# Stage 2 of a fused attention and feed-forward kernel: gate and value products by Strassen's method

## The chip, the cores and the metric

The kernel runs on one core of one Trainium2 chip. The metric is the device time of one execution in microseconds (us), as the median of several runs; lower is better.

## What is computed

Three layers in a row, all in 32-bit floats:

```python
attn_out = _attn_ref(q, k, v, n_global, n_local)       # 2 batches, 8 heads, 768 tokens, 64 per head
x = attn_out.transpose(0, 2, 1, 3).reshape(1536, 512)
h = x @ w_in                                           # 512 to 1024
solu = h * softmax(h)
y = (solu - mean) / sqrt(var + 1e-6) * g_ln @ w_out    # 1024 to 512
xn = y / sqrt(mean(y * y) + 1e-6) * rms_g
g, val = xn @ w_gate, xn @ w_val                       # 512 to 1536, each
out = (g / (1 + exp(-g)) * val) @ w_down               # 1536 to 512
```

The attention looks at 8 global keys and at the 96 keys before each query. The last three lines are stage 2.

## The kernel before, in words

**Precision.** Each matrix product is made of three matmuls (`product`, L412 to L415): every operand is split into a rounded part `hi` (ACT rounds it by a copy) and a rest `lo` (DVE subtracts), and hi*hi, hi*lo and lo*hi are summed in PSUM. So each weight and each activation costs one instruction on ACT and one on DVE besides the matmuls.

**Attention and first feed-forward.** The 1536 tokens go in 12 tiles of 128 (`one_tile`, t from -1 to 11), each with four slots p = 0 to 3, one for each pair of heads. Each engine runs its own hand-written list of one tile after another (PE from L1371, ACT from L762, DVE from L1129, POOL from L647, SP from L508), and the order on an engine is the order in which these functions call the operations. Semaphores tie the lists together. While tile t+1 is attended, tile t runs through `ffn_in` in slots 1 and 2, and tile t-1 is normalised: DVE takes the variance at slot 0 of the next tile (`take_variance`, L1059), POOL works out the inverse root by ten tiny instructions, each waiting for the last (`newton`, L582), DVE applies it at slot 1 (`apply_norm`, L1077), and PE turns the result at slot 2 (`turn_ln`, L1297) and multiplies by `w_out` (`ffn_out`, L1311). ACT copies y out and squares it (`copy_y`, L713), and SP stores it to a spill buffer in HBM (L438).

**Stage 2.** Tokens go in 6 blocks of 256 in the outer loop, and each block passes all 1536 hidden columns in 12 steps m of 128. All weights of stage 2 lie split in SBUF for the whole stage. A block's y is loaded (`load_y`, L442), scaled by an inverse root from POOL (`newton_y`, L604; DVE L1088 and L1103), turned on PE (`turn_y`, L1325), and split by ACT and DVE (L723, L1112). In a step (`one_step`, L1412) PE makes a gate product and a value product (`widen`, L1342: 4 k x 3 matmuls of 128 x 256 each), then the down product of the step before (`narrow`, L1355: 2 x 3 matmuls of 128 x 512), which is summed over all 12 steps in two PSUM banks. ACT takes the SiLU and rounds, DVE multiplies and splits (L735, L741, L1121, L1126). After the last step of a block ACT copies the two banks out and SP stores them (`copy_out`, L743; `store_out`, L453).

**Around the seam.** The weights of stage 2 are brought in and split by a table of slots (L399 to L408) while the last tiles are attended. After tile 11 PE does the rest of `ffn_out` of tile 10, three steps of stage 2 with `turn_ln` of tile 11 between them, and then all of `ffn_out` of tile 11 (L1459 to L1468). POOL's list there is `newton(t)` for every tile, with `newton_y(0)` after `newton(8)` and the others at the end (L647 to L654).

## Time and profile before

| what | value |
|---|---|
| median of 3 runs | 592.25 us (591.99 to 592.34) |
| the profiled execution, its own time | 591.57 us |
| span of its profile, first to last instruction | 589.8 us |
| TensorE clock granted, mean over the span | 0.991 of full |
| PE busy in the span | 558.5 us (95%), 3697 matmuls |
| DVE, ACT, POOL busy | 307.1, 265.5, 93.9 us |

PE is TensorE, DVE is VectorE, ACT is ScalarE, POOL is GpSimd, SP is SyncE, which issues the DMAs here. A matmul's shown duration is longer than its distance to the next one, since matmuls overlap in the array: prices of a matmul are taken from start to start. Lines "L..." are lines of the kernel before.

### The profile page before, as it was taken

To read this page: it belongs to the slowest core of one execution; us is meant where nothing else is said; L and a number is where in the kernel's file an instruction comes from. 1 tells how busy PE (TensorE), PEld (TensorE's weight loads), DVE (VectorE), ACT (ScalarE), POOL (GpSimd) and SP (SyncE) were. 2 spreads that over 40 slices of the span, in tenths; PEclk is the share of its full clock that TensorE was granted. 3 is DMA by queue.
4 is the path that set the end of the run, shared out by engine and by line. 5 is a ranking of instruction groups with operands and counts; after the bars stand their busy time and mean duration, and the time that the engine had idled before them with its cause. 6 is when DMAs were issued, how large, how long until landed. Compare 5 with 4: busy or idle time off the path is not lost.

```text
span 589.8 us, 10771 instructions
## 1 busy us (share of the span) xinstructions
PE 558.5 (95%) x3697; PEld 480.2 (81%) x3697; DVE 307.1 (52%) x790; ACT 265.5 (45%) x610; POOL 93.9 (16%) x223
## 2 busy tenths in 40 slices
PE   2786999999999999999999999999999999999997
PEld 1564777777777777768899999999999999999996
DVE  4769878877887898767465132222212222222221
ACT  3668666776677786746443212222221222222112
POOL 4541122124202223323000010000001000000000
PEclk9997999999999999999999999999999999999999
DMA  8656662444244422414340200020020000001000
GB/s 216 193 148 183 198 174 77 125 125 125 76 125 125 127 76 76 159 57 176 111 170 9 73 1 1 1 72 0 1 72 0 0 0 36 0 0 37 1 1 36
DMA packets 21613, 46.95 MB, mean 80 GB/s; under 512 B 2764, under 2 KB 2776, under 8 KB 21576
## 3 DMA queue, kind: packets, MB, share of 16 engines
q1 hardware_dynamic: 21264, 46.47, 26.2%
q8 instruction: 20, 0.33, 0.2%
q14 instruction: 17, 0.14, 0.1%
q10 hardware_dynamic: 312, 0.01, 0.0%
HBM read 40.18 MB, written 6.29 MB: 79 GB/s over the span
## 4 chain that ended last, share of the span: by engine, by line
PE 80%; DVE 10%; POOL 4%; issue 3%; ACT 1%; DMA 1%; ACTq 0%; DVEq 0%; SPq 0%
PE hidden L413 9%; PE hidden L414 8%; PE hidden L415 8%; PE mixed L1265 3%; PE turned L413 3%; PE turned L414 3%; PE mixed L413 3%; PE scores_a L413 3%; PE mixed L414 3%; PE scores_b L413 3%; PE scores_a L414 3%; PE scores_b L414 3%; PE scores_b L415 3%; PE scores_a L415 3%; PE turned L415 3%
## 5 line engine op out<-in xcount | busy, mean ns | idle before, releaser
L741 ACT ACTIVATE act_hi<-act_sb 128x256 fp32r<-128x256 f32 x72 | 30.2, 420 | 108.8 <-DVE act_sb L1121 108.8
L1121 DVE TENSOR_TENSOR act_sb<-mixed,silu 128x256 f32<-128x256 f32 x36 | 15.3, 425 | 94.1 <-PE mixed L415 93.9
L1121 DVE TENSOR_TENSOR act_sb<-turned,silu 128x256 f32<-128x256 f32 x36 | 15.3, 424 | 88.6 <-PE turned L415 85.9
L413 PE MATMUL hidden<-down_hi,act_hi 128*128 128x512 f32 x144 | 56.9, 395 | 0.1
L414 PE MATMUL hidden<-down_lo,act_hi 128*128 128x512 f32 x144 | 56.9, 395 | 0.0
L415 PE MATMUL hidden<-down_hi,act_lo 128*128 128x512 f32 x144 | 56.7, 394 | 0.0
L685 ACT ACTIVATE probs_t<-turned 116x512 f32<-116x512 f32 x48 | 28.7, 598 | 54.9 <-PE turned L1250 54.9
L1126 DVE TENSOR_TENSOR act_lo<-act_sb,act_hi 128x256 fp32r<-128x256 f32 x72 | 30.6, 426 | 35.0 <-ACT act_hi L741 35.0
L675 ACT ACTIVATE probs<-logits,neg_max 128x232 f32<-128x232 f32 x96 | 45.8, 481 | 6.0 <-DVE neg_max L1008 6.0
L413 PE MATMUL hidden<-in_hi,xt_hi 128*128 128x512 f32 x96 | 42.8, 446 | 0.9 <-DVE xt_lo L1031 0.5
L413 PE MATMUL turned<-yt_hi,val_hi 128*128 128x256 f32 x144 | 40.8, 283 | 0.0
L413 PE MATMUL mixed<-yt_hi,val_hi 128*128 128x256 f32 x144 | 40.8, 283 | 0.0
L413 PE MATMUL scores_a<-yt_hi,gate_hi 128*128 128x256 f32 x144 | 40.4, 281 | 0.0
L414 PE MATMUL turned<-yt_lo,val_hi 128*128 128x256 f32 x144 | 40.4, 280 | 0.0
L414 PE MATMUL mixed<-yt_lo,val_hi 128*128 128x256 f32 x144 | 40.4, 280 | 0.0
L414 PE MATMUL scores_b<-yt_lo,gate_hi 128*128 128x256 f32 x144 | 40.4, 280 | 0.0
L414 PE MATMUL scores_a<-yt_lo,gate_hi 128*128 128x256 f32 x144 | 40.3, 280 | 0.0
L415 PE MATMUL turned<-yt_hi,val_lo 128*128 128x256 f32 x144 | 40.3, 280 | 0.0
L415 PE MATMUL scores_b<-yt_hi,gate_lo 128*128 128x256 f32 x144 | 40.3, 280 | 0.0
L415 PE MATMUL scores_a<-yt_hi,gate_lo 128*128 128x256 f32 x144 | 40.3, 280 | 0.0
L413 PE MATMUL scores_b<-yt_hi,gate_hi 128*128 128x256 f32 x144 | 40.3, 280 | 0.0
L415 PE MATMUL mixed<-yt_hi,val_lo 128*128 128x256 f32 x144 | 40.3, 280 | 0.0
(147 smaller groups left out, 1540.2 us busy)
## 6 DMA issues: line engine op xcount, KB each, us to landing
qk_raw<-qk_pairs SPq DMA_DIRECT2D x96, 180.0 KB, 3.2
v_in<-v_windows SPq DMA_DIRECT2D x12, 448.0 KB
staging<-w_gate SPq DMA_DIRECT2D x3, 1024.0 KB, 7.4
staging<-w_val SPq DMA_DIRECT2D x3, 1024.0 KB, 5.8
y_spill<-y_out SPq DMA_DIRECT2D x12, 256.0 KB, 3.9
staging<-w_down SPq DMA_DIRECT2D x3, 1024.0 KB, 5.9
y_in<-y_spill SPq DMA_DIRECT2D x6, 512.0 KB, 3.9
out<-o_sb SPq DMA_DIRECT2D x12, 256.0 KB, 2.1
```

The costliest lines, as they stand in the source:

```text
L413: pe.matmul(acc, hi, other_hi, start=first, stop=False)
L414: pe.matmul(acc, hi, other_lo, start=False, stop=False)
L415: return pe.matmul(acc, lo, other_hi, start=False, stop=last)
L675: nc.scalar.activation(probs[:, p % 2, h], logits[:, 2 * (p % 2) + h], ACT.Exp, bias=neg_max[:, even, head:head + 1], scale=-1.0, accum_ou ...
L685: nc.scalar.activation(probs_t[:, p % 2], turned[0:HALF, :], ACT.Copy).then_inc(probs_t_ready, 1)
L741: nc.scalar.activation(act_hi[:, slot], act_sb[:, slot], ACT.Copy).then_inc(act_rounded, 1)
L1121: nc.vector.tensor_tensor(act_sb[:, slot], val_ps[slot][:, 0:WIDE], silu[:, slot], ALU.mult).then_inc(act_ready, 1)
L1126: nc.vector.tensor_tensor(act_lo[:, slot], act_sb[:, slot], act_hi[:, slot].bitcast(F32), ALU.subtract).then_inc(act_split, 1)
L1265: ins = pe.matmul(mixed[h * d:(h + 1) * d, p * P:(p + 1) * P], v_in[:, even, half, head * d:(head + 1) * d], probs_t[:, p % 2, h, half], s ...
```

## The change

Stage 2 is laid out anew. The weights go in 6 groups j of 256 hidden columns in the outer loop, and each group passes 3 blocks b of 512 tokens: 18 steps. Gate and value weights of a group, cut in two over the 512 inputs, form a matrix of 2 x 2 blocks, and so do the inputs of a block (halves of the 512 inputs, halves of the 512 tokens). Their product by Strassen's method (in Winograd's form) takes 7 block products, P1 to P7, where the plain way takes 8. A block product is 2 x 2 x 3 matmuls of 128 x 256. For it sums of weight blocks and sums of input blocks are formed (4 POOL additions per group, `sum_w`, and 4 per block, `sum_y`), each of the 7 factors is rounded and split (ACT, DVE; `round_w`, `split_w`, `round_y`, `split_y`), and the seven results are combined in 3 ACT copies, 2 POOL additions and 5 DVE additions per step. All 7 split factors of all three blocks of inputs stay in SBUF, so all tokens are turned and split during the last tiles and the first group. The inputs are now scaled by `rms_g` as they leave PSUM (`scale_y`, 4 ACT instructions of 128 x 128 per tile), and the weights are not. The down product of a step (`narrow`, 4 x 2 x 3 matmuls of 128 x 512) no longer stays in PSUM over a block's steps: DVE adds each result into `out_acc` in SBUF (`add_out`), and SP stores a tile of it once the last group is added.

Of the lists: y tiles 0 to 4 are turned in tiles 7, 8 and 11; POOL has `newton_y(0)`, `newton_y(1)` after `newton(5)`, `newton_y(2)` after `newton(6)`, `sum_y(0)` after `newton(7)`, `newton_y(3)` and `sum_w(0)` between `newton(9)` and `newton(10)`, and `newton_y(4)` ahead of `newton(11)`. The three weight blocks that were rounded and split in tiles 8 to 11 go out of those lists. The loops over tiles are now written out from t = 6. The core of the diff:

```diff
...
-    WIDE = 2 * P
+    doubles = tiles // 2
+    TOKENS = 4 * P
+    blocks = tiles // 4
+    HALF_T = TOKENS // 2
...
+    PRODUCTS = 7
+    P1, P2, P6, P5, P7, P4, P3 = range(PRODUCTS)
+    ADD_1, ADD_2, ADD_3, ADD_4 = range(1, 5)
...
+    T_ORDER = (P1, P2, P3, P7, P5, P6, P4)
...
+        turn_at = {(7, 0): 0, (7, 1): 1, (8, 0): 2, (8, 1): 3, (11, 3): 4}
+        round_y_at = {(8, 2): 0, (8, 3): 1, (9, 0): 2, (9, 1): 3, (9, 2): 4, (9, 3): 5, (10, 0): 6}
+        split_y_at = {divmod(pairs * t + p + 1, pairs): i for (t, p), i in round_y_at.items()}
+        round_w_at = {(11, 0): (0, 1, 2, 3), (11, 2): (4, 5, 6)}
+        split_w_at = {(11, 0): (0, 1, 2, 3), (11, 3): (4, 5, 6)}
+        NORMALISE_AT = {(6, 3): 0, (7, 3): 1, (10, 3): 2, (11, 2): 3}
+        SCALE_AT = {(6, 0): 0, (6, 3): 1, (7, 3): 2, (10, 3): 3, (11, 3): 4}
...
+            def load_w(j):
+                if is_first(j):
+                    sp.wait_ge(yt_split, PRODUCTS)
+                else:
+                    sp.wait_ge(w2_split, PRODUCTS * j)
+                for m, w in enumerate((w_gate, w_val)):
+                    sp.dma_start(w_raw[:, m], w.rearrange("(k p) n -> p k n", p=P)[:, :, bass.ds(j * FF, FF)]
+                                 ).then_inc(w2_loaded, 16)
...
+            def store_out(q):
+                sp.wait_ge(out_added, (groups - 1) * tiles + q + 1)
+                sp.dma_start(out_tiles[q], out_acc[:, q]).then_inc(out_stored, 16)
...
+                if known(t) and t == 10:
+                    load_w(0)
+                if known(t) and t == 11:
+                    load_y(3)
...
+            load_y(4)
+            load_down(0)
+            load_w(1)
             store_y(tiles - 2, 0)
-            for c in range(9, len(plan)):
-                load_block(sp, c)
-                if c == 10:
-                    store_y(tiles - 1, 1)
-            with sp.Fori(0, blocks // 2 - 1) as i:
-                for even in range(2):
-                    load_y(2 * i + (even + 2), even)
-                    store_out(2 * i + even)
-            for b in range(blocks - 2, blocks):
-                store_out(b)
...
+                g1, g2, v1, v2 = w_raw[:, 0, 0:2], w_raw[:, 0, 2:4], w_raw[:, 1, 0:2], w_raw[:, 1, 2:4]
+                at = 4 * j
+                pool.wait_ge(w2_loaded, 32 * (j + 1))
+                if known(j) and j == 1:
+                    pool.wait_ge(yt_split, 2 * PRODUCTS)
+                pool.tensor_tensor(added[:, 0], g1, v1, ALU.subtract).then_inc(w2_summed, 1)
+                pool.wait_ge(w2_summed, at + ADD_1)
+                pool.tensor_tensor(v1, v1, v2, ALU.add).then_inc(w2_summed, 1)
+                pool.wait_ge(w2_summed, at + ADD_2)
+                pool.tensor_tensor(added[:, 1], v1, g1, ALU.subtract).then_inc(w2_summed, 1)
+                pool.wait_ge(w2_summed, at + ADD_3)
+                pool.tensor_tensor(added[:, 2], g2, added[:, 1], ALU.subtract).then_inc(w2_summed, 1)
...
             for t in range(tiles):
+                if t == tiles - 1:
+                    newton_y(4)
                 newton(t)
                 if t % 2 == 0 and t + 4 < tiles:
                     set_bias(t + 4)
-                if t == tiles - 4:
+                if t == 5:
                     newton_y(0)
-            for b in range(1, blocks):
-                newton_y(b)
+                    newton_y(1)
+                if t == 6:
+                    newton_y(2)
+                if t == 7:
+                    sum_y(0)
+                if t == 9:
+                    newton_y(3)
+                    sum_w(0)
+            def one_step(j, b, more):
+                s = blocks * j + b
+                pool.wait_ge(corner_added, CORNERS * s + SUM_U2)
+                pool.wait_ge(partial_copied, COPIES * s + COPY_5)
+                pool.tensor_tensor(partial[:, 1], partial[:, 1], partial[:, 0], ALU.add).then_inc(middle_added, 1)
+                pool.wait_ge(partial_copied, COPIES * s + COPY_7)
+                pool.tensor_tensor(partial[:, 2], partial[:, 2], partial[:, 0], ALU.add).then_inc(middle_added, 1)
+                if more and b == 1 and not is_first(j):
...
+            sum_y(1)
+            one_step(0, 0, True)
+            newton_y(5)
+            one_step(0, 1, True)
+            sum_y(2)
+            sum_w(1)
+            one_step(0, 2, True)
+            for b in range(blocks):
...
+            def scale_y(tt):
+                act.wait_ge(yt_ready, tt + 1)
...
+                b, at = tt // 4, tt % 4 * P
+                for k in range(KM):
+                    ins = nc.scalar.activation(yt_raw[b][:, k, at:at + P], turned_x[:, k * P:(k + 1) * P], ACT.Copy,
+                                               scale=rms_col[:, k:k + 1])
+                ins.then_inc(yt_scaled, 1)
...
+            def one_step(j, b, more):
+                s = blocks * j + b
+                ahead = more and b == blocks - 1
+                if b == 1:
+                    round_down(j)
+                copy_1(s)
+                for i in (P1, P2) if ahead else ():
+                    round_w(j + 1, i)
+                take_silu(s, 0)
+                if ahead:
+                    round_w(j + 1, P6)
+                copy_5(s)
+                if ahead:
+                    round_w(j + 1, P5)
+                copy_7(s)
+                for i in (P7, P4) if ahead else ():
+                    round_w(j + 1, i)
+                round_act(s, 0)
+                take_silu(s, 1)
+                if ahead:
+                    round_w(j + 1, P3)
+                round_act(s, 1)
...
+            def sum_u2(s):
+                dve.wait_ge(product_ready, PRODUCTS * s + P6 + 1)
+                nc.vector.tensor_tensor(partial[:, 0], product_ps[P6][:], partial[:, 0], ALU.add
+                                        ).then_inc(corner_added, 1)
...
+            def add_out(j, b, i):
+                done = tiles * j + 4 * b + i
+                dve.wait_ge(down_ready, done + 1)
+                if is_first(j):
+                    nc.vector.tensor_copy(out_acc[:, 4 * b + i], o_ps[i % 2]).then_inc(out_added, 1)
+                    return
+                dve.wait_ge(out_added, done - tiles + 1)
+                nc.vector.tensor_tensor(out_acc[:, 4 * b + i], o_ps[i % 2], out_acc[:, 4 * b + i], ALU.add
+                                        ).then_inc(out_added, 1)
...
+            def one_step(j, b, more):
+                s = blocks * j + b
+                ahead = more and b == blocks - 1
+                before = (j, b - 1) if b > 0 else (j - 1, blocks - 1)
+                split_act(s - 1, 1)
+                if b == 0:
+                    split_w(j, P4)
+                    split_w(j, P3)
+                if b == 1:
+                    split_down(j)
+                gate_1(s)
+                for i in (P1, P2) if ahead else ():
+                    split_w(j + 1, i)
+                sum_u2(s)
+                for i in (P6, P5) if ahead else ():
+                    split_w(j + 1, i)
+                val_2(s)
+                add_out(*before, 0)
+                if ahead:
+                    split_w(j + 1, P7)
+                add_out(*before, 1)
+                val_1(s)
+                gate_value(s, 0)
+                gate_2(s)
+                split_act(s, 0)
+                add_out(*before, 2)
+                gate_value(s, 1)
+                add_out(*before, 3)
...
-            for half in range(2):
-                split_block(dve, OVER_ATTENTION, half)
-            for m in range(EARLY):
-                if m == EARLY - 1:
-                    apply_norm(tiles - 1)
-                one_step(0, m, 0)
+            gate_1(0)
+            apply_norm(tiles - 1)
+            sum_u2(0)
+            normalise_y(4)
+            split_y(1, 0)
             split_ln(tiles - 1, 0)
...
+            def widen(j, b, i):
+                s = blocks * j + b
+                if is_first(j):
+                    pe.wait_ge(yt_split, PRODUCTS * b + 1 + max(T_ORDER.index(e) for e in range(i + 1)))
+                if b == 0:
+                    pe.wait_ge(w2_split, PRODUCTS * j + i + 1)
...
+                if i == P1 and not first:
+                    pe.wait_ge(corner_added, CORNERS * (s - 1) + VAL_2)
+                    pe.wait_ge(partial_copied, COPIES * (s - 1) + COPY_7)
+                if i == P2 and not first:
+                    pe.wait_ge(corner_added, CORNERS * (s - 1) + VAL_1)
+                if i == P6 and not first:
+                    pe.wait_ge(corner_added, CORNERS * (s - 1) + GATE_2)
+                if i == P5 and not first:
+                    pe.wait_ge(partial_copied, COPIES * (s - 1) + COPY_5)
+                if i == P7:
+                    pe.wait_ge(partial_copied, COPIES * s + COPY_1)
+                if i == P4:
+                    pe.wait_ge(corner_added, CORNERS * s + GATE_1)
+                if i == P3:
+                    pe.wait_ge(corner_added, CORNERS * s + SUM_U2)
+                for f in range(2):
+                    cols, here = slice(f * P, (f + 1) * P), slice(f * HALF_T, (f + 1) * HALF_T)
+                    for k in range(2):
+                        ins = product(pe, product_ps[i][:, here], w7_hi[:, i, k, cols], w7_lo[:, i, k, cols],
+                                      yt_hi[b][:, i, k], yt_lo[b][:, i, k], k == 0, k == 1)
+                ins.then_inc(product_ready, 1)
...
+            def narrow(j, b, i):
+                s = blocks * j + b
+                half, cols = i // 2, slice(i % 2 * P, (i % 2 + 1) * P)
+                pe.wait_ge(act_split, 2 * s + half + 1)
...
+                    pe.wait_ge(out_added, 4 * s + i - 1)
+                for f in range(2):
+                    ins = product(pe, o_ps[i % 2], act_hi[:, half, f, cols], act_lo[:, half, f, cols],
+                                  down_hi[:, f], down_lo[:, f], f == 0, f == 1)
...
+            def one_step(j, b):
+                before = (j, b - 1) if b > 0 else (j - 1, blocks - 1)
+                for i in (P1, P2, P6, P5, P7):
+                    widen(j, b, i)
+                narrow(*before, 0)
+                narrow(*before, 1)
+                widen(j, b, P4)
+                widen(j, b, P3)
+                narrow(*before, 2)
+                narrow(*before, 3)
...
+            ffn_out(tiles - 2, range(4, 6))
+            turn_y(5)
+            ffn_out(tiles - 2, range(6, 8))
+            turn_y(6)
+            widen(0, 0, P1)
+            turn_y(7)
+            widen(0, 0, P2)
+            widen(0, 0, P6)
+            widen(0, 0, P5)
             turn_ln(tiles - 1, 0)
-            one_step(0, EARLY, 0)
+            widen(0, 0, P7)
             turn_ln(tiles - 1, 1)
-            ffn_out(tiles - 1, range(K1))
-            for m in range(EARLY + 1, M2):
-                one_step(0, m, 0)
-            with pe.Fori(0, (blocks - 2) // 2) as i:
-                for odd in range(2):
-                    for m in range(M2):
-                        one_step(2 * i + (1 + odd), m, 1 - odd)
-            for m in range(M2):
-                one_step(blocks - 1, m, 1)
-            narrow(blocks - 1, M2 - 1)
+            widen(0, 0, P4)
+            ffn_out(tiles - 1, range(0, 4))
+            turn_y(8)
+            ffn_out(tiles - 1, range(4, 8))
+            widen(0, 0, P3)
+            widen(0, 1, P1)
+            turn_y(9)
+            for i in (P2, P6, P5, P7):
+                widen(0, 1, i)
+            turn_y(10)
+            narrow(0, 0, 0)
+            turn_y(11)
+            narrow(0, 0, 1)
+            widen(0, 1, P4)
+            widen(0, 1, P3)
+            narrow(0, 0, 2)
+            narrow(0, 0, 3)
+            one_step(0, 2)
+            for b in range(blocks):
+                one_step(1, b)
+            with pe.Fori(2, groups - 1) as j:
+                for b in range(blocks):
+                    one_step(j, b)
+            for b in range(blocks):
+                one_step(groups - 1, b)
+            for i in range(4):
+                narrow(groups - 1, blocks - 1, i)
...
```

## Rows read from the trace of the kernel before

**Rows 1.** Busy time, from the page's first part (share of the span, instructions).

```profile
PE 558.5 (95%) x3697; PEld 480.2 (81%) x3697; DVE 307.1 (52%) x790; ACT 265.5 (45%) x610; POOL 93.9 (16%) x223
```

**Rows 2.** Windows: span, then busy us (instructions) of PE, PEld, DVE, ACT, POOL; PEclk, DMA.

```profile
290.00:390.00 100.00, 99.99 (x717) 93.68 (x716) 34.14 (x72) 31.69 (x68) 4.68 (x24) 1.00 0.16 57
```

**Rows 3.** Timeline of PE in stage 2: start us, duration us, instruction.

```profile
288.49 0.28 PE L413 MATMUL scores_b<-yt_hi,gate_hi 128*128 128x256 f32 x1
...
340.21 0.28 PE L413 MATMUL scores_b<-yt_hi,gate_hi 128*128 128x256 f32 x1
...
343.01 0.40 PE L413 MATMUL hidden<-down_hi,act_hi 128*128 128x512 f32 x1
...
344.40 0.28 PE L413 MATMUL scores_a<-yt_hi,gate_hi 128*128 128x256 f32 x1
```

**Rows 4.** Instruction groups of all engines: count | busy us, mean ns | idle before.

```profile
L413 PE MATMUL turned<-yt_hi,val_hi 128*128 128x256 f32 x144 | 40.8, 283 | 0.0
...
L735 ACT ACTIVATE silu<-scores_a 128x256 f32<-128x256 f32 x36 | 13.8, 383 | 57.4 <-PE scores_a L415 57.4
...
L1115 DVE TENSOR_TENSOR yt_lo<-turned_x,yt_hi 128x512 fp32r<-128x512 f32 x12 | 8.2, 684 | 0.4 <-ACT yt_hi L727 0.4
...
L1339 PE MATMUL turned_x<-ident,yn 128*128 128x128 f32 x48 | 7.2, 273 | 0.1
...
L1109 DVE TENSOR_SCALAR yn<-y_in,rstd 128x512 f32<-128x512 f32 x12 | 5.3, 481 | 0.0
...
L580 POOL COPY bias_even<-bias 128x1856 f32<-128x1856 f32 x3 | 5.6, 1877 | 5.0 <-DVE neg_max L1008 5.0
...
L643 POOL TENSOR_TENSOR in_lo<-staging,in_hi 128x1024 fp32r<-128x1024 f32 x2 | 4.7, 2389 | 8.4 <-ACT in_hi L373 8.4
```

**Rows 5.** Timeline of ACT at tile 9, slot 2.

```profile
224.11 0.60 ACT L711 ACTIVATE ln_hi<-turned_x 128x512 fp32r<-128x512 f32 x1 [1.24 <-PE turned_x L1308]
```

**Rows 6.** Timeline of POOL: `newton_y(0)`, then `newton(10)`.

```profile
222.47 0.20 POOL L613 TENSOR_TENSOR rstd<-rstd_bits 128x2 f32<-128x2 f32 x1
...
224.82 0.20 POOL L613 TENSOR_TENSOR rstd<-rstd 128x2 f32<-128x2 f32 x1
...
225.93 0.20 POOL L613 TENSOR_TENSOR rstd<-rstd 128x2 f32<-128x2 f32 x1
...
227.21 0.35 POOL L619 TENSOR_TENSOR rstd<-rstd 128x2 f32<-128x2 f32 x1
...
254.62 0.71 POOL L591 TENSOR_SCALAR col<-seed_bits,col 128x1 f32<-128x1 f32 x1 [12.46 <-DVE seed_bits L1074]
...
258.28 0.28 POOL L601 TENSOR_SCALAR col<-col 128x1 f32<-128x1 f32 x1
```

**Rows 7.** Timeline of DVE around the same `newton(10)`.

```profile
249.03 0.43 DVE L1020 COPY recip_wide<-recip 128x512 f32<-128x512 f32 x1
...
258.60 0.81 DVE L1079 TENSOR_SCALAR gated<-gated,moments,col 128x1024 f32<-128x1024 f32 x1 [3.48 <-POOL col L601]
```

**Rows 8.** Timeline of PE: `turn_ln` of tiles 10 and 11.

```profile
259.47 0.66 PE L1308 MATMUL turned_x<-ident,gated 128*128 128x128 f32 x4 [0.98 <-DVE gated L1079]
...
277.91 0.66 PE L1308 MATMUL turned_x<-ident,gated 128*128 128x128 f32 x4 [0.70 <-DVE gated L1079]
```

**Rows 9.** Windows early in attention, columns as in the second group.

```profile
50.00:55.00 5.00, 2.75 (x18) 1.93 (x20) 4.94 (x12) 4.62 (x11) 0.00 (x0) 0.66 0.90 249
55.00:60.00 5.00, 3.60 (x16) 2.83 (x15) 4.82 (x17) 3.19 (x8) 3.25 (x5) 0.50 0.30 84
60.00:65.00 5.00, 5.00 (x30) 3.95 (x29) 3.32 (x8) 2.77 (x7) 2.06 (x6) 0.82 0.49 144
```

**Rows 10.** DMA issues: count, KB each, median us from issue to landing.

```profile
y_in<-y_spill SPq DMA_DIRECT2D x6, 512.0 KB, 3.9
```

**Rows 11.** Timeline of the end.

```profile
584.34 0.19 PEld L413 LDWEIGHTS hidden<-down_hi,act_hi 128*128 128x128 f32 x1 [0.54 <-DVE act_lo L1126]
...
586.04 1.09 ACT L748 ACTIVATE o_sb<-hidden 128x512 f32<-128x512 f32 x2 [2.21 <-PE hidden L415]
```

619 lines of the change are left out of this document (367 added, 252 removed).

## The prediction

> **What bounds the kernel now.** The first view is busy time: PE is busy for 95% of the span, DVE for 52%, ACT for 45% [rows 1]. The second is the same by stretches: in 100 us of stage 2 PE is busy for 99.99, DVE for 34, ACT for 32 and POOL for 5, at full clock [rows 2]. So stage 2 lasts as long as its matmuls take one after another, and 1 us of PE work less there is 1 us less of time, as long as nobody makes PE wait. The third view gives their prices from start to start. From the first gate matmul of a step to the down product that follows are 24 matmuls of 256 columns: 2.80 us, 0.117 each; the six of 512 columns after it take 1.39 us, 0.232 each [rows 3]. Over the stage: from 288.49 [rows 3] to 584.34 [rows 11] are 69 steps, 10 sets of four transposes (0.35 each by their 273 ns and overlap [rows 4]) and a wait of some 0.3, so a step is (295.85 - 3.5 - 0.3) / 69 = 4.23 us, and 256 columns are (4.23 - 6 x 0.231) / 24 = 0.1185 us. Last I read the seam at tile 10 and 11, where PE does wait: `turn_ln` sits behind DVE, and DVE behind POOL's `newton` [rows 7, 8].
>
> **What the change takes away.** Before: 72 steps x 24 = 1728 matmuls of 256 columns and 432 of 512. After: 18 steps x 7 x 12 = 1512 and 432. Gone are 216 x 0.1185 = **25.6 us** of PE (25.2 at 0.117). A new step is 84 x 0.1185 + 24 x 0.231 = 15.5 us. Transposes are as many as before, and SP moves the same weights and the same y, so DMA is priced at nothing inside the stage: a group's 1 MB is asked for two steps, some 30 us, ahead.
>
> **What stands beside it in a step.** An instruction of 128x512 costs DVE 0.69 [rows 4] and ACT 0.60 [rows 5]; POOL's two-input operation cost 2.39 us for 1024 columns, so 1.2 for 512 [rows 4]. Per step DVE has 5 sums, 2 products, 2 splits of activations, 4 additions of output and a third of 9 weight splits: 16 x 0.69 = 11.0 us, in the third step of a group 18, 12.4 us. ACT has 7 and a third of 9: 10 x 0.6 = 6.0, at most 8.4. POOL has 2 and a third of 4: 4.0. All lie under 15.5. What each product waits for: P1 of the next step needs `val_2`, which hangs on P5, P7, one copy and POOL's addition, about 8.6 us into a step of 15.5. P6 of the next needs `gate_2`, ready 13.4 into the step and wanted at 18.3. The down products wait for splits that are one step old. The least slack is 3.7 us or more, so I cost the steady steps at nothing; what hides them is PE itself, and should DVE and POOL together take over 15.5, this cover is gone.
>
> **Tiles 6 to 10.** Four turns of y come in, with 4 ACT instructions of 128x128 each. The 256-column one costs 0.38 and the 512-column one 0.60 [rows 4, 5], so some 0.28, 1.1 us a tile. ACT sits idle for 1.24 us before `round_ln`, most of it while PE's transposes run [rows 5], and `turn_ln` must now wait for `scale_y` to free its bank: I take 0.5 us in tiles 7 and 8 each. DVE gains two scalings (0.9 us a pair [rows 4]) and loses weight splits. Together **+1.2** (0.2 to 3).
>
> **The seam, the largest cost.** In POOL's list `newton_y(3)` and `sum_w(0)` stand ahead of `newton(10)`, on which `apply_norm(10)`, `turn_ln(10)` and then all of PE wait. Before, `newton(10)` ran from 254.62 to 258.56 [rows 6], DVE waited 3.48 for it [rows 7] and PE 0.98, and the turn began at 259.47 [rows 8]. Now: `invert_sums` ends at 249.46 [rows 7]; `normalise_y(2)` and the three seed instructions of `scale_of_y(3)` follow, 0.9 + 0.6: 250.9. `newton_y(3)` has 12 instructions; four of them took 1.11 when nothing was beside them, the block of twelve 5.1 [rows 6]: 3.4 to 5.1, I take 3.4, since DVE works mostly on PSUM here. `sum_w(0)` is four dependent additions of 1.2 + 0.1: 5.1; up to four DVE instructions with both operands in SBUF (a split of x, three weight splits) fall beside it, and such neighbours stretched POOL's work in `newton_y(0)`, so 5.1 to 7.9, I take 6.9. Then `newton(10)`, 4.0 + 0.6 for the last splits, and 0.9 to the turn: 266.7. PE has nothing else in its list and stands still from 258.3 to there: **+7.3** (4.8 with all at the low ends; 11.6 at the high ends).
>
> A standstill of over 8 us has a second price. Early in attention PE was busy for 2.75 of 5 us, the clock fell to 0.66 and then 0.50, and in the next 5 us, fully busy, it was granted 0.82 on average [rows 9]: from the restart at 57.3 to full clock some 4.5 us went at half rate (1.2 GHz for 2.4). That loses **+2.2** (0 if the clock holds, 3.5 if it falls late and is slow to return).
>
> **After tile 11.** `newton_y(4)` stands ahead of `newton(11)`, but it can start 1.7 us after the last `ffn_in` and the seeds come at 6.1, so it hides; PE has 12.6 us of work there, and `apply_norm(11)` comes at about 13.0. I count waits of 0.5 there, 0.9 at the second `turn_ln` (behind `sum_u2`, a normalise and two splits on DVE), 0.3 before P6 of step 1, whose `gate_2` is queued behind ten DVE instructions, and 0.9 before `turn_y(10)`, since y of tile 11 must be stored and loaded again (3.9 us for a load [rows 10], about as much for a store). Gone is the 0.9 before `turn_ln(11)` [rows 8]. **+1.7** (0 to 6: in steps 1 and 2 DVE has up to 22 instructions, 15.2 us, with POOL beside it).
>
> **The end.** The last down products wait 0.54 less for `act_lo`, and one DVE addition of 0.69 takes the place of two ACT copies that last 1.09 [rows 11]: **-0.9** (-1.2 to 0).
>
> **The sum** is made against the profiled execution: 591.57 - 25.6 + 1.2 + 7.3 + 2.2 + 1.7 - 0.9 = 577.5. The median of the runs lies 0.7 above it: **578.2 us**. All terms at their low ends give 570.5, at their high ends 590.8.
>
> **A rule weighed.** What the rows show: POOL's same scalar step lasts longer when DVE has two SBUF operands beside it. The Trainium skill, page "SBUF — State Buffer", section "Who interferes with whom", says that such a DVE instruction and a GpSimd instruction that reads SBUF exclude each other, and that one with a single SBUF input does not. By it 7 of DVE's 16 instructions of a step shut out POOL and 9, those with an operand in PSUM, do not; in a steady step both would still end inside 15.5, and the seam would come near 7.3. No run here shows it for additions of this size.
>
> **Rivals.** *A cheap seam (0.15).* POOL's additions may cost what its copy cost, 1.88 us for 1856 columns [rows 4], 0.5 for 512. Then `sum_w(0)` takes 2.4, PE stops for 3 us, the clock stays: +2.1 for the seam, +1.2 after it, +0.8 in the tiles: 569.9. For it: nothing but the copy; against it: the subtraction of two operands was measured on this engine at 2.39 for 1024. *A jam in steps 0 to 2 (0.19).* DVE's list is over-full there, and each late `gate_2` or `val_1` stops PE: all 6 us after the seam and 2 to 3 more in it: about 584 to 588. For it: 15.2 us of DVE in 15.5; against it: PE's list has 12 us of other work between. *Slower (0.04).* DVE and POOL shut each other out in every step: 16 x (0.69 + 0.1 for each wait) + 4.0 = 16.6 us, 1.1 over PE's, 17 times 19 us: 597. It decides from 16.3 us per step on. For it: both lists are fuller than any in the trace of stage 2. Against it: nine of DVE's 16 instructions read PSUM, and the products that wait have 3.7 us in hand. A last 0.02 is for an end at no change.
>
> **How the numbers follow.** The forecast has 0.60: 578.2, with its own range 572 to 585. The range of 8 in 10 reaches down to the cheap seam and up into the jam: 569 to 586. A measurement of this kernel can tell about 0.2%, 1.2 us, from no change. Faster: 0.60 + 0.15 + 0.19 = 0.94; the same 0.02; slower 0.04.
>
> **What would show it.** In the changed profile: 1512 matmuls of 256 columns in stage 2, three steps of a group in 46.5 us with PE without a wait; a wait of 7 to 9 us of PE before `turn_ln` of tile 10 with POOL's `newton(10)` named behind it, and some 4 us of lower clock after it; short waits before P6 of step 1 and `turn_y(10)`. It is wrong if PE waits in the steady steps, if the additions on POOL take 0.5 or over 2 us, or if the wait at tile 10 is under 4 us.

## The result and the profile after

The changed kernel takes 586.75 us (median of 6 runs, 585.89 to 588.81), the kernel before on the same chips 592.30: ratio 0.9918, 95% interval 0.9896 to 0.9939. It is faster, by 5.5 us; the forecast was 14.1, and 586.75 lies 0.75 above the upper end of the range. The profiled execution took 586.26 us, its span is 584.2, its mean granted clock 0.977 (before 0.991).

The busy times, which answer to [rows 1]:

```profile
PE 540.1 (92%) x3481; PEld 462.7 (79%) x3481; DVE 439.1 (75%) x913; ACT 302.8 (52%) x661; POOL 191.5 (33%) x295
```

The 216 matmuls fewer are there (3697 to 3481). PE is 18.4 us less busy and idle for 44.1 us in place of 31.3. The busy time of DVE went from 307 to 439 us, that of POOL from 94 to 192. The same by stretches of ten microseconds around the seam, and 100 us of the steady steps (columns as in [rows 2]):

```profile
260.00:270.00 10.00, 4.06 (x17) 2.68 (x15) 6.81 (x8) 3.54 (x8) 9.01 (x13) 0.86 0.25 79
270.00:280.00 10.00, 8.54 (x37) 6.96 (x38) 6.17 (x13) 5.23 (x12) 1.73 (x10) 0.79 0.00 0
...
290.00:300.00 10.00, 7.22 (x41) 6.67 (x40) 9.13 (x12) 6.43 (x12) 6.59 (x5) 0.83 0.20 74
...
320.00:330.00 10.00, 6.52 (x40) 5.83 (x40) 9.90 (x10) 5.50 (x10) 9.62 (x6) 0.94 0.01 2
330.00:340.00 10.00, 10.00 (x67) 9.53 (x66) 8.81 (x13) 4.02 (x7) 3.06 (x3) 0.89 0.00 0
...
370.00:470.00 100.00, 100.00 (x699) 93.51 (x698) 73.07 (x104) 38.03 (x65) 30.43 (x23) 1.00 0.11 32
```

From 340 us on nothing is left to explain: PE is busy for 100.0 of 100 at full clock, and from one step's P5 to the next's are 15.49 us on average (forecast 15.5). What is missing lies ahead of 340, but for 0.2 us at the end. Between 250 and 340 four stretches of ten microseconds show a clock below 0.9, where the kernel before has 1.00 in every one. PE's waits, the five groups that the change made or lengthened most (us in total, times, longest):

```profile
PE turned_x L1618 <- DVE gated L1294: 6.8, 1, 6.8
PE scores_a L1546 <- DVE qk_hi L1199: 5.3, 6, 1.4
PE turned L461 <- DVE yt_lo L1328: 3.5, 1, 3.5
PE turned_x L1618 <- DVE ln_lo L1299: 2.8, 1, 2.8
PE turned_x L1618 <- ACT staging L860: 1.8, 2, 0.9
```

Three of these waits in PE's timeline, with the first matmuls behind the first one. The first answers to [rows 8], where PE waited 0.98 us before `turn_ln` of tile 10; the second stands before the second turn of tile 11, the third before product P6 of step (0, 2) (weight group 0, block 2). The 0.70 of [rows 8] before the first turn of tile 11 is gone:

```profile
271.34 1.12 PE L1618 MATMUL turned_x<-ident,gated 128*128 128x128 f32 x4 [6.83 <-DVE gated L1294]
272.11 0.78 PE L461 MATMUL hidden<-in_hi,xt_hi 128*128 128x512 f32 x1
272.69 0.63 PE L462 MATMUL hidden<-in_lo,xt_hi 128*128 128x512 f32 x1
273.11 0.63 PE L463 MATMUL hidden<-in_hi,xt_lo 128*128 128x512 f32 x1
...
294.59 1.12 PE L1618 MATMUL turned_x<-ident,gated 128*128 128x128 f32 x4 [2.78 <-DVE ln_lo L1299]
...
329.06 0.58 PE L461 MATMUL turned<-yt_hi,w_hi 128*128 128x256 f32 x1 [3.48 <-DVE yt_lo L1328]
```

The matmuls of 512 columns start 0.42 to 0.58 apart behind the standstill (a "stand" from here on), where 0.23 is the distance at full clock. The granted clock of 271:276 is 0.69, so a part of it ran at 1.2 GHz.

POOL's timeline, with what the forecast called `sum_w(0)` and `newton(10)` (the two lines of the latter answer to [rows 6]):

```profile
259.56 1.30 POOL L735 TENSOR_TENSOR staging<-w_raw 128x512 f32<-128x512 f32 x1
260.94 1.62 POOL L737 TENSOR_TENSOR w_raw<-w_raw 128x512 f32<-128x512 f32 x1
262.63 1.63 POOL L739 TENSOR_TENSOR staging<-w_raw 128x512 f32<-128x512 f32 x1
264.34 1.60 POOL L741 TENSOR_TENSOR staging<-w_raw,staging 128x512 f32<-128x512 f32 x1
265.93 1.28 POOL L656 TENSOR_SCALAR col<-seed_bits,col 128x1 f32<-128x1 f32 x1
...
270.16 0.28 POOL L666 TENSOR_SCALAR col<-col 128x1 f32<-128x1 f32 x1
```

Four additions took 6.4 us (forecast 6.9), and `newton(10)` waited for them. DVE's timeline shows what the forecast's sum did not price:

```profile
287.84 1.57 DVE L1294 TENSOR_SCALAR gated<-gated,moments,col 128x1024 f32<-128x1024 f32 x1
289.32 0.68 DVE L1349 TENSOR_TENSOR partial<-turned,partial 128x512 f32<-128x512 f32 x1
289.92 2.34 DVE L1322 TENSOR_SCALAR y_in<-y_in,rstd 128x512 f32<-128x512 f32 x2
292.19 1.75 DVE L1328 TENSOR_TENSOR yt_lo<-y_raw,yt_hi 128x512 fp32r<-128x512 f32 x1
293.86 0.68 DVE L1299 TENSOR_TENSOR ln_lo<-turned_x,ln_hi 128x512 fp32r<-128x512 f32 x1
...
322.17 3.49 DVE L1328 TENSOR_TENSOR yt_lo<-out_acc,yt_hi 128x512 fp32r<-128x512 f32 x2
```

From 287.56 to 296.7 POOL adds without a pause. In that time `apply_norm` takes 1.57 us (0.81 in [rows 7]), the two halves of a normalisation 2.34 (0.88 for such a pair at 274.33), a split of y 1.75 (0.69 elsewhere), and the two at 322.17 take 3.49. Operations between them that read PSUM, `sum_u2` at 289.32 and the split from `turned_x` at 293.86, keep their 0.68.

### The profile page after: what moved, and what is told of

It reads as the page before. It is cut to its first block, busy times and chain, and to the rows that moved or that the text cites. A ratio compares the mean times of both kernels' runs of the same rounds, so it can differ in the third digit from the quotient of the medians.

```text
span 584.2 us, 10751 instructions
## 1 busy us (share of the span) xinstructions
PE 540.1 (92%) x3481; PEld 462.7 (79%) x3481; DVE 439.1 (75%) x913; ACT 302.8 (52%) x661; POOL 191.5 (33%) x295
## 4 chain that ended last, share of the span: by engine, by line
PE 74%; DVE 16%; issue 4%; POOL 3%; ACT 2%; DMA 1%; DVEq 0%; ACTq 0%; SPq 0%
PE hidden L461 9%; PE hidden L462 9%; PE hidden L463 9%; PE turned L461 3%; PE turned L463 3%; PE scores_b L461 3%; PE turned L462 3%; PE scores_b L462 3%; PE scores_b L463 3%; PE scores_a L462 3%; PE scores_a L461 3%; PE scores_a L463 3%; PE mixed L1574 3%; PE turned L1559 2%; PE y_acc L463 2%
## 5 line engine op out<-in xcount | busy, mean ns | idle before, releaser
L814 ACT ACTIVATE probs_t<-turned 116x512 f32<-116x512 f32 x48 | 28.6, 596 | 58.5 <-PE turned L1559 58.5
L461 PE MATMUL hidden<-down_hi,acts 128*128 128x512 f32 x144 | 56.5, 393 | 0.0
L462 PE MATMUL hidden<-down_lo,acts 128*128 128x512 f32 x144 | 56.5, 392 | 0.0
L463 PE MATMUL hidden<-down_hi,acts 128*128 128x512 f32 x144 | 56.3, 391 | 0.0
L1386 DVE TENSOR_TENSOR out_acc<-hidden,out_acc 128x512 f32<-128x512 f32 x60 | 41.3, 688 | 9.6 <-PE hidden L463 8.7
L461 PE MATMUL turned<-yt_hi,w_hi 128*128 128x256 f32 x144 | 41.3, 286 | 3.5 <-DVE yt_lo L1328 3.5
L461 PE MATMUL scores_b<-yt_hi,w_hi 128*128 128x256 f32 x144 | 41.4, 287 | 0.0
L463 PE MATMUL turned<-yt_hi,w_lo 128*128 128x256 f32 x144 | 41.1, 285 | 0.0
L462 PE MATMUL turned<-yt_lo,w_hi 128*128 128x256 f32 x144 | 41.1, 285 | 0.0
L463 PE MATMUL scores_b<-yt_hi,w_lo 128*128 128x256 f32 x144 | 41.0, 285 | 0.0
L462 PE MATMUL scores_b<-yt_lo,w_hi 128*128 128x256 f32 x144 | 41.0, 285 | 0.0
L461 PE MATMUL scores_a<-yt_hi,w_hi 128*128 128x256 f32 x144 | 40.7, 283 | 0.0
```

The source lines that it names most:

```text
L461: pe.matmul(acc, hi, other_hi, start=first, stop=False)
L462: pe.matmul(acc, hi, other_lo, start=False, stop=False)
L463: return pe.matmul(acc, lo, other_hi, start=False, stop=last)
L814: nc.scalar.activation(probs_t[:, p % 2], turned[0:HALF, :], ACT.Copy).then_inc(probs_t_ready, 1)
L1386: nc.vector.tensor_tensor(out_acc[:, 4 * b + i], o_ps[i % 2], out_acc[:, 4 * b + i], ALU.add).then_inc(out_added, 1)
```

## The experiments

All start from the changed kernel unless said otherwise; the kernel before ran beside each batch, at 591.1 to 591.7. Theory A of each is the one I hold: the orders of the lists and the exclusion between DVE and POOL make the stands, and the stands make the clock fall. "Exclusion" means that an instruction of one of the two engines waits until one of the other has ended. **Where a difference to the changed kernel is given, it is that of the ratios times 592.** The brackets are 95% intervals of the ratio; the changed kernel's is [0.9896, 0.9939].

The runs of one kernel lie up to 5 us apart here, those of the kernel before within 1.8, so differences of 1 to 2 us between medians are not clear of noise by themselves. The traces show two parts that differ from execution to execution. One is the clock behind the first stand (experiment 2). The other lies ahead of everything that the experiments change: the reciprocals' turn of tile 7 starts between 170.12 and 172.10 us, and an early wait of PE for POOL's `in_lo` goes from none to 1.9 us. So small differences are read below from distances inside the traces.

**1. `sum_w(0)` behind `newton(10)`.**

```
-                if t == 9:
-                    newton_y(3)
-                    sum_w(0)
+                if t == 9:
+                    newton_y(3)
+                if t == 10:
+                    sum_w(0)
-        round_w_at = {(11, 0): (0, 1, 2, 3), (11, 2): (4, 5, 6)}
-        split_w_at = {(11, 0): (0, 1, 2, 3), (11, 3): (4, 5, 6)}
+        round_w_at = {(11, 0): (0, 1), (11, 2): (2, 3, 4, 5, 6)}
+        split_w_at = {(11, 0): (0, 1), (11, 3): (2, 3, 4, 5, 6)}
```

> POOL's list holds sum_w(0) (four additions, 6.4 us in the trace) behind newton(10) in place of ahead of it; the roundings of the sums are moved with it. Nothing else changes. Theory A (the order of POOL's list makes the stand of 6.83 us before turn_ln of tile 10, and the stand makes the clock fall): newton(10) starts right behind newton_y(3), at about 259.6 in place of 265.9, the wait before turn_ln is 0.5 to 1 us, the granted clock of that stretch stays above 0.95 and 579 to 581 us come out, 6 to 7.5 under the changed kernel. Rival B (the stand is only handed on: the additions then end late, the roundings and splits of the weights crowd ACT and VectorE in tile 11, and PE waits there instead): the wait before turn_ln shrinks as well, but a new one of 3 to 6 us stands at the first or second product of step (0, 0), and the time is 584 to 587 us.

582.59 us (580.71 to 585.75), ratio 0.9864 [0.9826, 0.9902], 3.2 us less. The time lies between the two theories. B's new wait of 3 to 6 us in step (0, 0) did not come, only one of 0.84 before the first turn of tile 11, and the second turn waits 3.04. A's size is missed too: the wait went from 6.83 to 3.18, not to 1.

```profile
267.21 1.11 PE L1619 MATMUL turned_x<-ident,gated 128*128 128x128 f32 x4 [3.18 <-DVE gated L1295]
```

The order of POOL's list is worth 3.65 us of the wait. `newton(10)` itself took 4.96 us beside two splits on DVE (4.0 in [rows 6]), and `apply_norm` 1.74 beside `sum_w(0)`, which now began just before it. The clock still fell, to 0.83 in 260:270.

**2. The stand filled with work that nobody reads.**

```
+                    if known(t) and t == tiles - 1 and p == 2:
+                        pe.wait_ge(logits_ready, heads * tiles)
+                        pe.wait_ge(probs_t_ready, pairs * tiles)
+                        for _ in range(26):
+                            pe.matmul(scores[0][:], xt_hi[:, even, 0], w_hi["in", 0][:, 0], start=True, stop=True)
                     if p == 2 and is_tile(t - 1):
                         turn_ln(t - 1, 0)
```

> 26 dependence-free products of 128x512 (about 6.1 us at 0.233 each), whose result nobody reads, stand on TensorE just ahead of turn_ln of tile 10, inside the stand of 6.83 us. POOL's list is as in the changed kernel, so turn_ln starts when it did. Theory A: the clock does not fall in the stretch behind it, the matmuls of 0.31 to 0.43 us spacing at 272 to 274 go back to 0.23, and the kernel is 1.3 to 2.2 us faster than the changed one although it does more work: that is the price of the clock by itself. Rival B (the fall has nothing to do with the stand): the clock of 270:280 stays at about 0.8 and the time is within 0.5 us of the changed kernel.

585.63 us (584.83 to 586.74), ratio 0.9901 [0.9884, 0.9917]: 1.0 us less, with 26 matmuls more. That is under A's 1.3 to 2.2, and the interval overlaps that of the changed kernel, so the profile decides; its windows:

```profile
262.00:272.00 10.00, 9.30 (x39) 7.04 (x38) 6.37 (x6) 2.71 (x6) 8.59 (x14) 1.00 0.22 79
272.00:282.00 10.00, 9.28 (x47) 7.30 (x48) 7.55 (x18) 6.48 (x13) 2.35 (x12) 1.00 0.00 0
```

The clock stays at 1.00 here, so the fall hangs on the stand, and B falls. From the turn to the first matmul of P5 of step (0, 0) are 16.01 us. In the changed kernel these are 17.04. Of the six other experiments that leave this stretch alone (4, 5, 6, 7, 10, 11) one has 17.04 and five have 17.8 to 18.0. So the fall behind the first stand costs 1.0 to 2.0 us, not the same in every execution.

**3. The kernel before, with a late `newton(10)`.**

```
+                if t == tiles - 2:
+                    for i in range(4):
+                        pool.wait_ge(seed_ready if i == 0 else extra, tiles - 1 if i == 0 else i)
+                        pool.tensor_tensor(rel_i[:].bitcast(F32), key_i[:].bitcast(F32), key_i[:].bitcast(F32), ALU.add
+                                           ).then_inc(extra, 1)
                 newton(t)
```

> The kernel before, with four additions of 128x464 on POOL between the seed of tile 10 and newton(10), whose result nobody reads; about 1.2 us each, 4.8 to 5.8 together. It measures what a late newton(10) costs where nothing of Strassen's method is there. Theory A: the wait before turn_ln of tile 10, 0.98 us in the kernel before, grows by the whole length of the additions to about 6, the clock falls in the ten microseconds behind it, and the time is 592.3 + 5.5 + 1.5 = 598 to 600 us. Rival B (later tiles take the delay up: TensorE has other work that closes the gap): under 3 us of it reach the end, 593 to 595 us.

597.26 us (597.03 to 597.57), ratio 1.0102 [1.0085, 1.0119], 6.15 more than the 591.11 beside it. The four additions took 4.45 us and the wait grew from 0.98 to 5.03; PE's timeline:

```profile
262.75 1.12 PE L1314 MATMUL turned_x<-ident,gated 128*128 128x128 f32 x4 [5.03 <-DVE gated L1085]
```

and the windows behind it:

```profile
262.00:267.00 5.00, 4.25 (x15) 3.57 (x15) 3.91 (x6) 0.60 (x1) 0.00 (x0) 0.50 0.00 0
263.00:268.00 5.00, 5.00 (x17) 4.13 (x17) 2.96 (x6) 1.19 (x2) 0.00 (x0) 0.50 0.00 0
```

Of the 6.15 us 4.05 are wait, which leaves 2.1 for the clock of 0.50 (1.2 GHz) over five microseconds and more. The traces agree: from the turn to the first matmul into `mixed` are 17.05 us here and 14.80 in the kernel before, 2.25 more. No later tile takes any of it up: B falls. This is the seam's step of the forecast, in a kernel without any of Strassen's method.

**4. DVE's list: the splits of the layer norm first.**

```
-            normalise_y(4)
-            split_y(1, 0)
             split_ln(tiles - 1, 0)
-            split_y(1, 1)
+            normalise_y(4)
+            split_y(1, 0)
             split_ln(tiles - 1, 1)
+            split_y(1, 1)
```

> VectorE's list behind tile 11: the two splits of the last layer norm go ahead of normalise_y(4), split_y(1, 0) and split_y(1, 1). Theory A (the 2.78 us before the second turn_ln are the four operations ahead of the split in VectorE's list, two of them stretched beside POOL's additions): the wait shrinks to below 0.5 us, the clock does not fall in 290:300, and the time is 2 to 4 us under the changed kernel, 583 to 584.5. Rival B (the split is only traded: y's normalisation and splits come later by as much, and turn_y(8) or the first product of step (0, 1) waits for them): the sum of the waits of 285:312 stays at 2 to 3 us and the time within 1 us of the changed kernel.

586.51 us (586.50 to 588.17), ratio 0.9920 [0.9903, 0.9936]: no difference. The wait of 2.78 is gone from the second `turn_ln`, and this stands in its place:

```profile
307.43 0.63 PE L1645 MATMUL turned_x<-ident,y_in 128*128 128x128 f32 x4 [2.73 <-ACT out_acc L860]
```

`turn_y(9)` waits for ACT's `scale_y(8)`, which stands in ACT's list behind `round_act(0, 0)`, whose input DVE now delivers later. Rival B was right: 2.78 became 2.73.

**5. `sum_w(1)` early.**

```
             one_step(0, 0, True)
+            sum_w(1)
             newton_y(5)
             one_step(0, 1, True)
             sum_y(2)
-            sum_w(1)
```

> POOL's list alone: sum_w(1), four additions, stands ahead of newton_y(5), where POOL is idle from 297 to 306, in place of behind sum_y(2), where it runs from 323.4 to 330.1. Theory A (in the changed kernel the 3.48 us before product P6 of step (0, 2) are VectorE's splits of y, and these are late because POOL's additions shut VectorE's operations with two inputs in SBUF out: two splits took 3.49 and two 2.84 where two take 1.3 elsewhere): behind 323.4 the splits go back to 0.6 to 0.7 each, the wait falls below 1 us, and the time is 2.5 to 4 us under the changed kernel, 583 to 584.3. Rival B (the splits are late by VectorE's own list, not by POOL): the splits stay where they are or gain under 0.5 us, and the time is within 1 us of the changed kernel.

584.98 us (584.69 to 586.51), ratio 0.9897 [0.9877, 0.9917], 1.2 us less; the intervals overlap. The wait before P6 of step (0, 2) fell from 3.48 to 1.44 and its fall of clock is gone (1.00 in 320:340); 0.89 is new at `turn_y(10)`. Two pairs of splits of y took 2.38 and 1.28 us in place of 3.49 and 2.84, so 2.04 of the 3.48 us came with `sum_w(1)` beside them. From P5 of step (0, 0) to P5 of step (1, 0) the trace is 1.8 us shorter. That is half or less of A's size: `sum_y(2)` still stands beside the first pair.

**6. DVE's list unchanged, POOL held back.**

```
-            sum_y(1)
+            pool.wait_ge(ln_split, N1 * tiles - 1)
             one_step(0, 0, True)
+            sum_y(1)
```

> POOL's list alone, around the second turn_ln of tile 11: POOL waits for the first split of the last layer norm, then makes the two additions of step (0, 0), then sum_y(1). VectorE's list is that of the changed kernel, the same operations in the same order; they only run without POOL beside them. Theory A (exclusion): apply_norm takes 0.81 again in place of 1.57, the two halves of normalise_y(4) 0.88 in place of 2.34 together, split_y(1, 0) 0.68 in place of 1.75; the split is done 2 to 2.8 us sooner, the wait of 2.78 falls below 0.6, and if the sums of y, 5.6 us later than they were, are still in time for the products of step (0, 1), the time is 2 to 3.8 us under the changed kernel. Rival B (as with the order of VectorE's list in the run before: what is won here is lost at the next wait): the later sums of y and the later val of step (0, 0) make a new wait of 2 us and more at turn_y(9) or in step (0, 1), and the time is within 1 us of the changed kernel.

587.58 us (587.56 to 588.70), ratio 0.9940 [0.9923, 0.9957]: if anything slower. This is the cleanest look at the exclusion, the same operations in the same order as in the fence of DVE above:

```profile
288.36 0.81 DVE L1295 TENSOR_SCALAR gated<-gated,moments,col 128x1024 f32<-128x1024 f32 x1
289.09 0.68 DVE L1350 TENSOR_TENSOR partial<-turned,partial 128x512 f32<-128x512 f32 x1
289.69 0.87 DVE L1323 TENSOR_SCALAR y_in<-y_in,rstd 128x512 f32<-128x512 f32 x2
290.48 0.68 DVE L1329 TENSOR_TENSOR yt_lo<-y_raw,yt_hi 128x512 fp32r<-128x512 f32 x1
```

and in PE's timeline:

```profile
306.54 0.75 PE L1646 MATMUL turned_x<-ident,y_in 128*128 128x128 f32 x4 [3.39 <-ACT out_acc L861]
```

0.81, 0.87 and 0.68 in place of 1.57, 2.34 and 1.75: with POOL silent they are as short as in attention, and the second `turn_ln` waits for nothing. A is shown as the mechanism, and B as the price: the sums of y begin at 295.16 in place of 287.56, 7.6 us later, ACT's roundings wait for them, `scale_y(8)` stands behind these, and PE waits 3.39 there.

**7. ACT's list: the scaling ahead of the exponentials.**

```
+                    if known(t) and t in (7, 8) and p == 1:
+                        scale_y(turn_at[t, p])
                     exp_pair(n + 1, 1 - even if p < pairs - 1 else even, (p + 1) % pairs)
...
-                    if known(t) and (t, p) in turn_at:
+                    if known(t) and (t, p) in turn_at and not (t in (7, 8) and p == 1):
                         scale_y(turn_at[t, p])
```

> ACT's list alone: in tiles 7 and 8 the second scale_y of the tile goes ahead of the two exponentials of that pair. In the changed kernel turn_ln waits 0.89 and 0.91 us for it. Theory A (a wait of TensorE of its own length, which nothing behind it takes up): both waits go, 1.4 to 1.8 us less, 585.0 to 585.4. Rival B (the exponentials, 1.1 us later, are waited for in its place): TensorE waits for the probabilities or for round_ln instead, and the time is within 0.4 us of the changed kernel.

584.83 us (584.03 to 585.77), ratio 0.9883 [0.9866, 0.9899], 2.1 us less. In the trace 1.6 are won by the last turn of reciprocals, which starts at 254.02 for 255.49, after a start of the stretch 0.1 later. Both waits of 0.9 are gone and nothing took their place: A. In attention these two waits, 1.8 us together, were worth nearly their own length.

**8. 1, 5, 6 and 7 together**, and `sum_w(0)` held until the norm of tile 10 is applied:

```
                 if t == 10:
+                    pool.wait_ge(ln_ready, t + 1)
                     sum_w(0)
```

> All orders together: sum_w(0) behind newton(10) and held until VectorE has applied the norm of tile 10, sum_w(1) ahead of newton_y(5), sum_y(1) behind the first split of the last layer norm and the additions of step (0, 0), and the scaling ahead of the exponentials in tiles 7 and 8. Theory A (the three standstills and the falls of the clock behind them are what stands between the forecast and the changed kernel): the waits of 6.83, 2.78 and 3.48 us shrink to about 2.3, 0.5 and 0.5, the falls of the clock go with them, and 570 to 574 us come out, 13 to 16 under the changed kernel. Rival B (the waits are the sign of VectorE being full in 255:335, 8 to 9.9 us of every 10; what is won at one is lost at the next): the time stays above 578 us.

580.28 us (578.61 to 580.80), ratio 0.9801 [0.9781, 0.9821], 6.9 us less: faster than either kernel, but 6 us short of A's range and inside B's (above 578). The first wait is 2.28, as expected, and the clock is 1.00 from 250 to 300. But the waits of 260:330 still add up to 10.2 us (13.5 in the changed kernel): 3.42 at `turn_y(9)`, 1.50 at P6 of step (0, 1), 1.44 at that of (0, 2), 1.06 at `turn_y(4)`. Behind the 3.42 the clock fell after all, to 0.66:

```profile
300.00:310.00 10.00, 7.68 (x44) 7.44 (x45) 8.38 (x12) 5.19 (x14) 7.15 (x15) 0.66 0.33 124
```

**9. Three moves more, for the waits of 3.42 and 1.50.** The edit in short: each engine's list in its new order, with a plus at the calls that moved ahead.

```
 ACT   for place in range(2, 6): round_y(1, place)
+ACT   copy_y(tiles - 1, 1); scale_y(8); copy_1(1)
 ACT   round_y(1, 6); round_down(0); round_act(0, 0)
 DVE   split_y(1, 4); split_y(1, 5)
+DVE   scale_of_y(5); gate_2(0)
 DVE   split_y(1, 6); split_down(0); split_act(0, 0)
 POOL  one_step(0, 0, True)
+POOL  newton_y(5)
 POOL  sum_w(1)
```

> The kernel with all orders together, with three moves more around step (0, 1): ACT copies y of tile 11 and scales its first part as soon as they are there, ahead of the last rounding of y, the rounding of the down weights and round_act(0, 0); VectorE takes scale_of_y(5) and gate_2(0) ahead of the last split of y, the split of the down weights and split_act(0, 0); POOL takes newton_y(5) ahead of sum_w(1). Theory A (the waits of 3.42 at turn_y(9) and 1.50 at product P6 of step (0, 1) are places in the lists of ACT and VectorE, and the granted clock of 0.66 in 300:310 comes from them): the first falls to about 0.5, the second goes, the clock stays above 0.9 in 290:310, and 574 to 576.5 us come out, 4 to 6 under the kernel before this one. Rival B (the load behind the lists is what is full, so another product waits): the sum of TensorE's waits from 285 to 330 stays above 4.5 us and the time above 578.5 us.

578.67 us (577.59 to 579.91), ratio 0.9775 [0.9755, 0.9795], 1.5 less than experiment 8; the intervals overlap, and the traces show 1.8 less from tile 7 to step (1, 0). Both waits went, and 4.08 came at `turn_y(10)`, behind DVE's `normalise_y(5)`, which took 2.29 beside `sum_w(1)`. The waits of 285:330 add up to 6.0 us, and the time stayed above 578.5: B. PE's timeline:

```profile
308.75 1.06 PE L1652 MATMUL turned_x<-ident,y_in 128*128 128x128 f32 x4 [4.08 <-DVE y_in L1328]
```

and DVE's:

```profile
306.40 2.29 DVE L1328 TENSOR_SCALAR y_in<-y_in,rstd 128x512 f32<-128x512 f32 x2
```

**10. A third of one block product left out** (`two_terms` is `product` without its second matmul):

```
-                        ins = product(pe, product_ps[i][:, here], ...)
+                        ins = (two_terms if i == P7 else product)(pe, product_ps[i][:, here], ...)
```

> The changed kernel without one of the three products of the pair of halves in block product P7 (the weights' high part by y's low part): the output lacks this term. 4 matmuls of 128x256 fewer in each of 18 steps, 72 in all, and everything else, the additions too, as it is. Theory A (the steps are bound by TensorE, a matmul of 256 columns is worth its 0.1185 us): 72 x 0.1185 = 8.5 us less, of which those in the first three steps may go into the waits there: 577.8 to 579.8 us, and steps of 15.02 in place of 15.49 us. Rival B (the steps are near the bound of VectorE, 71 to 73 per cent busy, and of the chain through ACT, POOL and VectorE from one product to the next use of its bank): the steps shrink by less than 0.3 us and the time stays above 581.5 us.

579.65 us (579.29 to 581.12), ratio 0.9806 [0.9787, 0.9825], 6.6 us less, inside A's range. The steady steps are 15.03 us from P5 to P5 (15.49 in the changed kernel), 0.116 for each of the four matmuls of 256 columns. 0.463 in each of 15 steps are 6.9, so the first three steps seem to give back next to nothing. The price under the main term of the forecast is confirmed within some 2%: 216 x 0.116 are 25.1 us.

**11. Two additions more in each steady step,** twice the step's own two. Both inputs of the new ones are the same tile; they took 1.12 us each, the step's own 1.29 to 1.36.

```
                 pool.tensor_tensor(partial[:, 2], partial[:, 2], partial[:, 0], ALU.add).then_inc(middle_added, 1)
+                if not known(j) or j >= 1:
+                    for i in range(2):
+                        ...
+                        pool.tensor_tensor(nowhere[:], quiet[:], quiet[:], ALU.add).then_inc(more_done, 1)
```

> Two additions of 128x512 more on POOL in each of the 15 steps of weight groups 1 to 5, behind the step's own two, whose result nobody reads: POOL's share in the steady steps goes from 27 to about 45 per cent. Theory A (the price of the additions in the steady steps is fully covered: TensorE is busy 220.0 of 220 us and the nearest chain has room): steps of 15.5 us as before and a time within 1 us of the changed kernel, though VectorE's operations with two inputs in SBUF (the split of acts, the gate by value) show stretched durations. Rival B (the exclusion makes them late enough to be waited for, as in steps 0 to 2): new waits of TensorE of 0.3 to 1 us in each step, and 591 to 600 us.

586.25 us (585.58 to 586.93), ratio 0.9905 [0.9889, 0.9922]: no difference, and steps of 15.49.

```profile
400.00:500.00 100.00, 100.00 (x697) 93.41 (x696) 72.93 (x105) 37.33 (x64) 43.40 (x34) 1.00 0.10 32
```

POOL is busy for 43 of 100 us and PE for 100.0. The exclusion is there too (a split of `acts` takes 0.77 on average for 0.73), and PE does not wait for it.

**12. One move more, for the wait of 4.08:** `normalise_y(5)` right behind the second gate by value, and POOL holds `sum_w(1)` for it:

```
             newton_y(5)
+            pool.wait_ge(yn_ready, 6)
             sum_w(1)
```

> The reordered kernel with two moves more: VectorE takes normalise_y(5) straight behind the second gate by value, ahead of split_act(0, 1), gate_1(1), a split of y and sum_u2(1), and POOL holds sum_w(1) until that normalisation is done. Theory A (the 4.08 us before turn_y(10) are again the place in VectorE's list and POOL's additions beside it, which stretched the two halves from 0.87 to 2.29): the wait shrinks to below 1 us, and 573.5 to 576 us come out. Rival B (the seam is now bound by the sum of what VectorE, ACT and POOL do there, so a later wait takes its place): another 2 us and more of waits stand between 305 and 330, and the time stays within 1.5 us of the reordered kernel's 578.7.

579.20 us (576.75 to 579.59), ratio 0.9774 [0.9754, 0.9795], the same as the kernel of 9. The 4.08 at `turn_y(10)` is gone, 2.43 stands at `turn_y(11)` and 2.41 before P6 of step (0, 2):

```profile
307.90 0.63 PE L1653 MATMUL turned_x<-ident,y_in 128*128 128x128 f32 x4 [2.43 <-ACT out_acc L864]
...
322.30 0.39 PE L461 MATMUL turned<-yt_hi,w_hi 128*128 128x256 f32 x1 [2.41 <-DVE yt_lo L1335]
```

B again. The kernels of 9 and 12 are the fastest of these runs, some 13 us under the kernel before.

## Why the prediction was wrong

The profiled execution against the sum, term by term; the forecast total was 577.5 on this scale, 586.26 came. None of the prediction's own signs of being wrong came: no wait in the steady steps, additions of 1.3 to 1.75 us, and a wait of 6.83 us at tile 10. The miss lies in two terms for which it had named no sign.

- **Matmuls gone: -25.6, as forecast** (25.1 at the 0.116 of experiment 10). The steps are 15.49 us, and 18 of them are 25.7 less than 72 of 4.23.
- **Steady steps covered: right.** No wait from 340 us on, and twice the additions cost nothing (experiment 11). The slower rival, exclusion in every step, is out.
- **Tiles 6 to 10: forecast +1.2 (0.2 to 3), measured +4.1, outside its range.** From the reciprocals' turn of tile 7 to that of tile 11 are 84.82 us where 79.27 were (170.67 to 255.49, before 170.88 to 250.15); four sets of transposes that came in from stage 2 are 1.4 of the 5.55. The two waits for `scale_y` that I took at 0.5 were 0.89 and 0.91, and they are worth nearly their length (experiment 7). Not foreseen were waits of 0.86, 0.88, 0.41 and 0.43 of `score_pair` for DVE's `qk_hi`, 2.6 together, none of which the kernel before has in these tiles. The trace shows what stands ahead of them: in tile 7 `normalise_y` and the seed of the next scale fill DVE's list from 171.56 to 173.13, so the splits for the scores end 1.4 us later in the tile; in tile 9 it is a split of y of 0.68. I had set these against weight splits that go, which do not go from these places. No experiment tests it.

```profile
171.56 0.88 DVE L1322 TENSOR_SCALAR y_in<-y_in,rstd 128x512 f32<-128x512 f32 x2
...
178.97 0.37 PE L1546 MATMUL scores_a<-qk_hi 128*128 128x232 f32 x1 [0.86 <-DVE qk_hi L1199]
...
219.20 0.68 DVE L1328 TENSOR_TENSOR yt_lo<-staging,yt_hi 128x512 fp32r<-128x512 f32 x1
```

- **The seam: forecast +7.3, measured +6.3.** 5.85 more before `turn_ln(10)` and 0.45 before the last `ffn_in`. The mechanism holds (experiments 1 and 3), and `sum_w(0)` took 6.4 us for the forecast 6.9. "PE has nothing else in its list" was right.
- **The clock behind it: forecast +2.2, measured 1.0** in this execution and up to 2.0 in others (experiment 2), 2.1 in experiment 3.
- **After tile 11: forecast +1.7 (0 to 6), measured 8.3. This is the step that failed.** I had 0.9 before the second `turn_ln` and 0.3 before P6 of step 1. It was 2.78 and, one step later, 3.48, less the 0.70 that went: 5.6. The 0.5 ahead of them and the 0.9 before `turn_y(10)` did not come. Behind each of the two stands the clock fell: the turn and the 12 matmuls of P4 took 3.46 us (1.92 in experiment 8, at full clock), those of P6 2.73 (1.52 in experiment 9): 1.5 and 1.2. The forecast had one stand and one fall; with the seam's there were three of each.
- **The end: -0.9 forecast, -0.7 measured** (the last matmul starts 3.5 us ahead of the span's end, 4.2 before).

Measured terms: 591.57 - 25.6 + 4.1 + 6.3 + 1.0 + 8.3 - 0.7 = 585.0; 1.3 us are not assigned. Against the forecast 6.6 us came more after tile 11 and 2.9 more in tiles 6 to 10; the seam and its clock came 2.2 cheaper.

Why that step failed: in [rows 6] I saw POOL's operations longer beside DVE's and raised POOL's prices for it. That DVE's operations grow as well I left out of DVE's sums; only the upper end of the term's range speaks of POOL beside them. There DVE has little room: 9.1, 8.7 and 9.9 us of ten in 290:300, 310:320 and 320:330, though only 5.9 in 300:310. What was left out, measured: `apply_norm` 0.81 with POOL silent and 1.57 beside an addition, a split of y 0.68 and 1.75, an operation with an operand in PSUM 0.68 both times (experiment 6 against the changed kernel). This stretching made all of the wait of 2.78 (experiment 6) and 2.04 of that of 3.48 (experiment 5). That it also made the stretch as a whole 6.6 us dearer is not shown: without it, in experiment 6, the kernel was not faster. On the rule weighed in the prediction: the Trainium skill, "SBUF — State Buffer", section "Who interferes with whom", says that the one who comes second is blocked for the whole instruction of the other, and it counts a `tensor_scalar` in a two-port mode among those that can contend. By that rule `apply_norm` and `normalise_y` may be caught too, though they have one tensor input, and the rows agree (0.81 to 1.57, 0.87 to 2.34). I had told the rule without these modes and had applied it to POOL's times alone.

The likeliest rival, the jam in steps 0 to 2 at 584 to 588, has the measured 586.75 in its range and named the place. It took 6 us after the seam, where 8.3 came, and 2 to 3 more in the seam, where it was cheaper: part of its agreement is luck.

What can be had back: the orders of the lists give 8.5 us, about as much as was missing, but not from where it was missing. Two distances in the traces, in us, show it; a start is that of the first matmul:

| kernel | reciprocals' turn of tile 7 to P5 of step (0, 0) | P5 of step (0, 0) to P5 of step (1, 0) |
|---|---|---|
| changed | 117.7 | 59.0 |
| 1 | 113.9 | 58.9 |
| 4 | 118.6 | 59.2 |
| 5 | 118.7 | 57.2 |
| 6 | 118.7 | 59.9 |
| 8 | 111.3 | 59.5 |
| 9 | 111.3 | 57.7 |
| 12 | 111.3 | 58.5 |

Experiments 2, 7 and 11 have 59.1 to 59.5 in the last column. Of the 7.8 us that the kernel of 9 wins in these two stretches, 6.4 lie ahead of P5 of step (0, 0): the stands before `turn_ln(10)` and in attention, taken away by 1 and 7. Behind it, where the forecast failed, no order wins more than 1.8. There 4, 6, 9 and 12 each removed the wait they were aimed at, and each time 2.4 to 4.1 us turned up at a later one. Whether a schedule exists that empties this stretch, or whether the work there must shrink, these runs leave open.

## What to carry to other kernels

The count of the work saved was right within half a microsecond. What was lost stood in the stretch from tile 7 to step (0, 2), in which the new form starts up and every engine makes its first weights, sums and splits. Price such a stretch with a list of its own for each engine, with both partners of an exclusion stretched, and look for a fall of the clock behind every long stand of the bound engine, not only behind the longest. Where an edit moves a wait and does not shorten the stretch, the next wait stands close behind: measure the whole stretch, and not the wait that the edit was aimed at. Whether taking work out would help more was not tried here.

## What the hardware showed that was not expected

- The exclusion is mutual. Two splits that take 1.29 together when POOL is silent took 3.48 to 3.49 beside additions, 1.1 us more for each, and the additions 1.59 to 1.75 where 1.28 is their time alone. One scalar step of `newton` on a single column, 0.34 us alone (experiment 3), took 1.74 beside splits (experiment 1).
- `apply_norm`, one tensor input in SBUF, is stretched as well (0.81 to 1.57, 1.74 or 1.77), and so are the halves of `normalise_y` (0.87 to 2.29 and 2.34 for a pair). `apply_norm` alone does 1024 columns in 0.81 us, 1.7 times the columns per us of a split.
- A stand of 2.78 us was followed by a fall of the clock (0.83 in 290:300), one of 2.28 (experiment 8) by none; in experiment 12, 2.43 and 2.41 were followed by 0.87 in 310:320 and 0.83 in 320:330. The fall behind the same stand of 6.8 us cost 1.0 us in some traces and 1.8 to 2.0 in others, in kernels that are alike in this stretch (experiment 2).
